# Fourier filter and two dense layers: one way-back matmul instead of two from the ninth group on, with an addition on VectorE and swaps and spreads on ScalarE

## The reference, cut to what matters

```python
X = np.fft.rfft(x, axis=1)                    # x: (2, 3008, 256)
Y = X * (filt_r + 1j * filt_i)[None]
y = np.fft.irfft(Y, n=3008, axis=1).reshape(6016, 256)
h = y @ w_in;  y = elu(h) @ w_out             # w_in (256, 2048), w_out (2048, 256)
h = y @ w2_in; y = (h * clip(h + 3, 0, 6) / 6) @ w2_out
```

## Time and profile before

| | before |
|---|---|
| median of three runs | 1123.72 (1123.43 to 1124.48) |
| the profiled execution's own time | 1124.28 |
| its span | 1122.5 |
| TensorE busy in the span | 1109.4 |
| VectorE, ScalarE, GpSimd busy | 733.0, 761.5, 291.3 |
| granted TensorE clock | 1.0 throughout |

### The profile page before, as it was taken

How to read it: one execution, slowest core, us unless ns; L and a number is a source line. 1 busy time by engine, 2 the same in 40 slices (tenths; PEclk the granted TensorE clock), 3 DMA queues, 4 the chain that set the end, 5 groups by cost and what they waited for, 6 DMA issues and landing times.

```text
span 1122.5 us, 13359 instructions
## 1 busy us (share of the span) xinstructions
PE 1109.4 (99%) x4842; PEld 890.1 (79%) x4842; DVE 733.0 (65%) x900; ACT 761.5 (68%) x1125; POOL 291.3 (26%) x228
## 2 busy tenths in 40 slices
PE   8999899999999999999999999999999999999998
PEld 4666678888888888888888888888888888888886
DVE  6777367566566667566677776666666666665665
ACT  0221588888888888888899766666665666665654
POOL 4876411102102102111269731111111120120000
PEclk9999999999999999999999999999999999999999
DMA  9887300100200200200311200200200101000000
GB/s 256 279 256 226 114 1 1 67 8 1 74 1 1 74 1 1 74 1 1 112 38 57 93 1 1 74 1 1 74 1 24 51 1 37 38 1 1 37 1 37
DMA packets 31185, 59.30 MB, mean 53 GB/s; under 512 B 3600, under 2 KB 19856, under 8 KB 31120
## 3 DMA queue, kind: packets, MB, share of 16 engines
q1 hardware_dynamic: 24784, 48.10, 13.2%
q10 hardware_dynamic: 6336, 10.36, 2.7%
HBM read 39.94 MB, written 18.51 MB: 52 GB/s over the span
## 4 chain that ended last, share of the span: by engine, by line
PE 88%; ACT 6%; DVE 4%; issue 2%; DMA 1%; POOL 0%; ACTq 0%
PE ps L384 41%; PE ps L373 12%; PE ps L375 12%; PE ps L374 12%; PE ps L337 3%; PE ps L312 2%; PE ps L328 2%; PE ps L329 2%; PE ps L320 2%; ACT e L491 2%; DVE e L611 2%; ACT e L493 1%; ACT ystage L485 1%; DMA f_ring<-f_dev 1%; ACT w_hi L467 1%
## 5 line engine op out<-in xcount | busy, mean ns | idle before, releaser
L616 DVE TENSOR_TENSOR g_lo<-e,g_hi 128x502 fp32r<-128x502 f32 (+1 forms) x288 | 277.1, 990 | 135.7 <-ACT g_hi L523 135.7
L373 PE MATMUL ps<-op_hi,w_hi 128*128 128x502 f32 x672 | 262.5, 391 | 2.8 <-ACT ps L518 1.7
L375 PE MATMUL ps<-op_lo,w_hi 128*128 128x502 f32 x672 | 261.8, 390 | 0.0
L374 PE MATMUL ps<-op_hi,w_lo 128*128 128x502 f32 x672 | 261.2, 389 | 0.0
L384 PE MATMUL ps<-g_lo,w_hi 128*128 128x502 f32 x768 | 237.4, 390 | 1.7 <-DVE g_lo L616 1.5
L384 PE MATMUL ps<-g_hi,w_hi 128*128 128x502 f32 x768 | 236.2, 389 | 0.0
L384 PE MATMUL ps<-g_hi,w_lo 128*128 128x502 f32 x768 | 235.6, 388 | 0.0
L682 POOL TENSOR_TENSOR op_lo<-op_raw,op_hi 128x1004 fp32r<-128x1004 f32 (+1 forms) x48 | 100.3, 2091 | 487.9 <-ACT op_hi L475 487.9
L384 PEld LDWEIGHTS ps<-g_lo,w_hi 128*128 128x128 f32 x768 | 143.6, 188 | 33.0 <-DVE g_lo L616 4.4
L384 PEld LDWEIGHTS ps<-g_hi,w_lo 128*128 128x128 f32 x768 | 144.5, 188 | 29.3
L384 PEld LDWEIGHTS ps<-g_hi,w_hi 128*128 128x128 f32 x768 | 144.1, 188 | 29.5 <-ACT g_hi L523 0.6
(11 more groups left out here) (51 smaller groups left out, 1149.8 us busy)
## 6 DMA issues: line engine op xcount, KB each, us to landing
f_ring<-f_dev SPq DMA_DIRECT2D x32, 384.0 KB, 4.4
op_raw<-y SPq DMA_DIRECT2D x36, 251.0 KB, 3.6
x_ring<-x_dev SPq DMA_DIRECT2D x32, 192.0 KB, 4.7
y<-ystage SPq DMA_DIRECT2D x12, 502.0 KB, 2.8
out_dev<-ystage SPq DMA_DIRECT2D x12, 502.0 KB, 2.8
y<-ystage ACTq DMA_DIRECT2D x24, 235.0 KB, 2.8
w_raw<-w_dev ACTq DMA_DIRECT2D x16, 256.0 KB, 4.3
w_raw<-w_dev SPq DMA_DIRECT2D x16, 256.0 KB, 3.1
```

Source lines behind the costliest of these rows:

```text
L373: pe.matmul(out, w_hi[p][:, cols], hi, start=start, stop=False, skip_group_check=True)
L374: pe.matmul(out, w_lo[p][:, cols], hi, start=False, stop=False, skip_group_check=True)
L375: pe.matmul(out, w_hi[p][:, cols], lo, start=False, stop=True, skip_group_check=True).then_inc(done, 1)
L616: return dve.tensor_tensor(g_lo[:, tiles, :], e[:, tiles, :], f32(g_hi[:, tiles, :]), ALU.subtract)
```

## The change

From group 8 on (`NZ`), the imaginary part of the product is no longer carried through a matmul of its own. ScalarE copies the two halves of `part_x` crosswise into a PSUM bank of its own (`swap_halves`, two copies of 64 partitions, bank 1). VectorE multiplies the swapped halves with the signed imaginary filter into `prod_i`, the straight ones with the real filter in place in PSUM, and adds both into `prod_r` (`combine`). One matmul with `I2` remains in `part_r`. The sign of the filter's imaginary part is turned on the host, and `I2J` with it, so that the first eight groups compute what they did. In every second of these groups (odd i) VectorE writes its transposition contiguously into `turned`, and ScalarE spreads it into `back` (`spread`). The inverse pieces have bank 0 alone, and behind the last group bank 2 in turn. TensorE makes `part_x(i + 1)` ahead of `part_a(i + 2)` from step 7 on. The ring of x has seven slots instead of eight; `turned` takes the space.

```diff
--- before.py
+++ after.py
@@ -30,9 +30,11 @@
 IJ = 5
 PIECES = (J + IJ - 1) // IJ
 NPIECE = len(ORDER) * PIECES
-XSLOTS = 8
+LAST_I = NPIECE - PIECES
+XSLOTS = 7
 FSLOTS = 3
 YSLOTS = 4
+NZ = GROUPS
 MATS = ("A", "BX", "I2", "I2J", "I1")
 
 
@@ -88,7 +90,7 @@
             m["BX"][c, 64 + k1], m["BX"][s, 64 + k1] = -si, co
             m["I2"][k1, c], m["I2"][64 + k1, c] = co, -si
             m["I2"][k1, s], m["I2"][64 + k1, s] = si, co
-    m["I2J"][0:64], m["I2J"][64:P] = m["I2"][64:P], -m["I2"][0:64]
+    m["I2J"][0:64], m["I2J"][64:P] = -m["I2"][64:P], -m["I2"][0:64]
     return np.stack([m[n] for n in MATS], axis=1).reshape(P, len(MATS) * P).astype(np.float32)
 
 
@@ -121,6 +123,7 @@
             spec = sbuf(fft, "spec", [P, 2, GCOL])
             prod_r = sbuf(fft, "prod_r", [P, 2, XCOL])
             prod_i = sbuf(fft, "prod_i", [P, 2, XCOL])
+            turned = sbuf(fft, "turned", [P, GCOL])
             back = sbuf(fft, "back", [P, 2, J, P])
         op_hi.append(sbuf(ctx, "op1_hi", [P, 7, T], F32R))
         with ExitStack() as raw:
@@ -140,7 +143,9 @@
             return mats[:, at:at + P]
 
         def ps_i(n):
-            return ps[:, n % 2, 0:IJ * ICOL]
+            return ps[:, 2 if n > LAST_I and (n - LAST_I) % 2 else 0, 0:IJ * ICOL]
+
+        ps_swap = ps[:, 1, 0:XCOL]
 
         def ps_a(i):
             return ps[:, 2 + i % 2, :]
@@ -167,6 +172,8 @@
         zeroed, pad_stored = sem("zeroed"), sem("pad_stored")
         a_done, x_done, r_done, i_done = sem("a_done"), sem("x_done"), sem("r_done"), sem("i_done")
         spec_ready, prod_ready, back_ready = sem("spec_ready"), sem("prod_ready"), sem("back_ready")
+        turn_done, spread_ready = sem("turn_done"), sem("spread_ready")
+        swap_ready, straight_ready, swapped_ready = sem("swap_ready"), sem("straight_ready"), sem("swapped_ready")
         signed = sem("signed")
         i_evac = sem("i_evac")
         y0_stored = [sem(f"y0_stored{k}") for k in range(YSLOTS)]
@@ -191,6 +198,13 @@
 
         def group_of(i):
             return ORDER[i // GROUPS], i % GROUPS
+
+        def direct(i):
+
+            return i < NZ or i % 2 == 0
+
+        def directs(n):
+            return sum(direct(i) for i in range(n))
 
         def piece_at(i):
 
@@ -322,17 +336,26 @@
 
             def part_r(i):
                 pe.wait_ge(prod_ready, i + 1)
-                if i >= 2:
-                    pe.wait_ge(back_ready, i - 1)
+                if i >= 2 and direct(i - 2):
+                    pe.wait_ge(back_ready, directs(i - 1))
+                elif i >= 2:
+                    pe.wait_ge(turn_done, i - 1 - directs(i - 1))
                 dst = ps_r(i)[:, :, 0:K2]
-                pe.matmul(dst, mat("I2"), prod_r[:, i % 2, :], start=True, stop=False)
-                pe.matmul(dst, mat("I2J"), prod_i[:, i % 2, :], start=False, stop=True).then_inc(r_done, 1)
+                if i < NZ:
+                    pe.matmul(dst, mat("I2"), prod_r[:, i % 2, :], start=True, stop=False)
+                    pe.matmul(dst, mat("I2J"), prod_i[:, i % 2, :], start=False, stop=True).then_inc(r_done, 1)
+                else:
+                    pe.matmul(dst, mat("I2"), prod_r[:, i % 2, :], start=True, stop=True).then_inc(r_done, 1)
 
             def part_i(n):
                 pos, j0, nj = piece_cols(n)
-                pe.wait_ge(back_ready, GROUPS * (pos + 1))
-                if n >= 2:
-                    pe.wait_ge(i_evac, n - 1)
+                pe.wait_ge(back_ready, directs(GROUPS * (pos + 1)))
+                if pos:
+                    pe.wait_ge(spread_ready, GROUPS * (pos + 1) - directs(GROUPS * (pos + 1)))
+                if n == LAST_I + 1:
+                    pe.wait_ge(spec_ready, NG - 1)
+                elif n:
+                    pe.wait_ge(i_evac, n - 1 if n > LAST_I else n)
                 for j in range(nj):
                     last = pe.matmul(ps_i(n)[:, j * ICOL:j * ICOL + ICOL], back[:, pos % 2, j0 + j, :],
                                      mat("I1")[:, 0:ICOL], start=True, stop=True)
@@ -353,10 +376,14 @@
             pe.wait_ge(zeroed, 4)
             part_r(0)
             for i in range(1, NG):
-                if i + 2 < NG:
+                if i + 1 < NZ:
                     part_a(i + 2)
-                if i + 1 < NG:
                     part_x(i + 1)
+                else:
+                    if i + 1 < NG:
+                        part_x(i + 1)
+                    if i + 2 < NG:
+                        part_a(i + 2)
                 part_r(i)
                 n = piece_at(i)
                 if n is not None:
@@ -494,10 +521,29 @@
                 else:
                     act.activation(dst, src, ACT.Relu, bias=3.0).then_inc(ready, 1)
 
+            def spread(i):
+                pos, g = i // GROUPS, i % GROUPS
+                act.wait_ge(turn_done, i + 1 - directs(i + 1))
+                if pos >= 2:
+                    act.wait_ge(i_done, PIECES * (pos - 1))
+                act.copy(back[:, pos % 2, :, g * GD:g * GD + GD],
+                         turned[:].rearrange("p (d j) -> p j d", j=J)).then_inc(spread_ready, 1)
+
+            def swap_halves(i):
+                act.wait_ge(x_done, i + 1)
+                if i > NZ:
+                    act.wait_ge(swapped_ready, i - NZ)
+                act.copy(ps_swap[0:64], ps_x(i)[64:P])
+                act.copy(ps_swap[64:P], ps_x(i)[0:64]).then_inc(swap_ready, 1)
+
             for i in range(NG + PIECES):
                 n = piece_at(i - 1) if i <= NG else None
                 if n is not None:
                     evac_piece(n)
+                if NZ <= i + 1 < NG:
+                    swap_halves(i + 1)
+                if 1 <= i <= NG and not direct(i - 1):
+                    spread(i - 1)
                 for p in range(PAIRS):
                     if i == w_step(p) - 2:
                         load_w(p)
@@ -583,13 +629,31 @@
                 dve.tensor_tensor(prod_i[:, i % 2, :], ps_x(i), f_ring[:, i % FSLOTS, 1, :],
                                   ALU.mult).then_inc(prod_ready, 1)
 
+            def combine(i):
+                dve.wait_ge(swap_ready, i - NZ + 1)
+                dve.wait_ge(signed, i + 1)
+                dve.wait_ge(prod_ready, i - 1)
+                dve.wait_ge(r_done, i - 1)
+                dve.tensor_tensor(prod_i[:, i % 2, :], ps_swap, f_ring[:, i % FSLOTS, 1, :],
+                                  ALU.mult).then_inc(swapped_ready, 1)
+                dve.wait_ge(f_loaded[i % FSLOTS], 16 * (i // FSLOTS + 1))
+                dve.tensor_tensor(ps_x(i), ps_x(i), f_ring[:, i % FSLOTS, 0, :], ALU.mult).then_inc(straight_ready, 1)
+                dve.wait_ge(swapped_ready, i - NZ + 1)
+                dve.wait_ge(straight_ready, i - NZ + 1)
+                dve.tensor_tensor(prod_r[:, i % 2, :], ps_x(i), prod_i[:, i % 2, :], ALU.add).then_inc(prod_ready, 1)
+
             def turn_r(i):
                 pos, g = i // GROUPS, i % GROUPS
                 dve.wait_ge(r_done, i + 1)
                 if pos >= 2 and g == 0:
                     dve.wait_ge(i_done, PIECES * (pos - 1))
                 dst = back[:, pos % 2, :, g * GD:g * GD + GD].rearrange("p j d -> p d j")
-                dve.transpose(dst, ps_r(i)).then_inc(back_ready, 1)
+                if direct(i):
+                    dve.transpose(dst, ps_r(i)).then_inc(back_ready, 1)
+                else:
+                    if directs(i) < i:
+                        dve.wait_ge(spread_ready, i - directs(i))
+                    dve.transpose(turned[:], ps[:, 6 + i % 2, :]).then_inc(turn_done, 1)
 
             dve.memset(back[:, 0, 0:4, :], 0.0).then_inc(zeroed, 1)
             dve.memset(pad_zero[:], 0.0).then_inc(zeroed, 1)
@@ -601,8 +665,10 @@
             for i in range(NG):
                 if i + 2 < NG:
                     turn_a(i + 2)
-                if i + 1 < NG:
+                if i + 1 < NZ:
                     products(i + 1)
+                elif i + 1 < NG:
+                    combine(i + 1)
                 turn_r(i)
 
             def second_act(u, src, ap, ready, done):
@@ -732,7 +798,7 @@
         rows = f[row].reshape(N1, K2, DH, GROUPS, GD).transpose(2, 0, 3, 4, 1)
         parts.append(np.concatenate([rows, rows], axis=1).reshape(DH, P, GROUPS, XCOL))
     f_dev = np.concatenate(parts, axis=3).transpose(0, 1, 2, 3)
-    sign_dev = np.concatenate([sgn, sgn], axis=0)
+    sign_dev = np.concatenate([-sgn, sgn], axis=0)
 
     def pieces(w_in, w_out):
         a = w_in.reshape(DH, P, PAIRS, 2, P).transpose(2, 1, 0, 3, 4)
```

## The result

The changed kernel takes 1126.95 us (median of 16 runs, 1124.13 to 1128.96) against 1123.99 of the kernel before: a ratio of 1.0024, 95% interval 1.0017 to 1.0031. It is slower by 3.0 us, where 1119.3 us was predicted. Its profiled execution is its fastest run, 1124.13, with a span of 1122.3.

A forecast was written before the change was run, and what follows sets the result against it. The weight-load ring was taken to bound the stage: 37.67 + 10.9 + 11.2 + 30.3 = 90.1 us, last X 110.4, tail 6.1, last pieces 116.5 not 120.89. 1124.28 - 4.4 = 1119.9 profiled, 1119.3 median; range 1113.0 to 1125.0.

The forecast's parts named there:

- The step that failed: Behind the start of the last pieces, pieces and dense layers keep their length, so the 4.4 us gain stays.
- the tail: From the last X product to the last seven pieces: 6.1 us, against 5.01 before, with pieces starting at 116.5.
- rival (c): Weight loads land slower as DMA has little room: 1126.3 us at 1.4 us more, 1129.3 at 2 more; chance 0.12.
- TensorE's step: In the transform stage, a step with a piece falls from 3.91 to 3.27 us without the second way-back matmul.
- VectorE: Its work per new-way group takes 2.85 us on the mean, under 3.27, so it does not bound piece steps.
- the swap: Two ScalarE copies from PSUM to PSUM, 466 ns each, 0.87 us for both, bounds 0.75 and 1.1.
- The spread: ScalarE's copy of 512 columns in SBUF: 0.62 us, 0.55 with overlap, 0.95 kept as the dearer case.
- rival (b): Copies and spreads on ScalarE are dearer, swap 1.1 us and spread 0.95: 1123.0 us; chance 0.18.
- The ring: Three-step loop of weight rounding, load issue, landing and GpSimd's sums sets the pace: 10.9, 11.2, then 10.1 us a block.
- Rival (a): TensorE sets the stage's pace and the ring costs nothing after block 2: 1113.4 us; chance 0.20.
- The block ends: In the one step of eight without a piece, VectorE becomes the bound, at 0.5 us each.
- The start: DMA-bound opening: one x slot less brings the rounding of block 2 forward 0.65 us, to 37.67.

The follow-up runs named there:

- e9: Changed kernel without spreads, last two groups the old way, and each weight load issued only after the swap ahead of it completed: 1117.19 us, ratio 0.9939.

## Why the prediction was wrong

**The step that failed** is the sentence that all behind the last pieces' start "has the same instructions and is carried along". The instructions are the same, but not their clock: 12.62 - 7.38 = 5.24 us on the last pieces and 3.21 - 1.88 = 1.33 on the four behind them, 6.6 us together. The waits that did it were in the sum: the tail was called "a chain with nothing beside it", its length was worked out, and the question of what an idle TensorE does was not put. None of the rivals had it. That the median lies near the 1126.3 us of rival (c) is chance.

For the profiled executions the sum closes. 1119.9 us was predicted and 1124.13 measured, 4.2 more: 6.6 of clock, less 1.4 because the last pieces started at 115.08 and not at 116.5, less 0.9 because from the first matmul of the dense layers to the end of the span it is 992.2 us, against 993.1 before. The prediction had named a change of this last length as a sign of its being wrong. It is not the change's: three other kernels here have 992.2 too (the one without spreads, the same with filled waits, and e9), the rest 993.0 to 993.4, and no run says why. The median lies 2.8 us above the profiled run, in part for the clock, as told above.

With the tail filled the changed kernel measured 1119.9, where 1119.3 was predicted. That is partly luck: the errors of the other steps, which follow, cancel in part, and in that kernel's trace the last pieces start at 117.45.

**TensorE's step, VectorE, the swap: right.** 3.27 us in piece steps, and VectorE below it. Its timeline in a step:

```profile
73.52 0.52 DVE L637 TENSOR_TENSOR prod_i<-ps,f_ring 128x384 f32<-128x384 f32 x1
73.96 0.56 DVE L640 TENSOR_TENSOR ps<-ps,f_ring 128x384 f32<-128x384 f32 x1
74.62 0.56 DVE L643 TENSOR_TENSOR prod_r<-ps,prod_i 128x384 f32<-128x384 f32 x1
75.10 0.71 DVE L656 STREAM_TRANSPOSE turned<-ps 128x512 f32<-128x512 f32 x1
```

From start to start it is 0.44 + 0.66 + 0.48 us. The addition waits for its own engine and starts 0.66 us after the product ahead of it, which is that product's 0.56 and 0.10 more: the upper bound of the prediction, where 0.60 was taken. Lines by form (busy us, mean ns, idle ahead of them):

```profile
L643 DVE TENSOR_TENSOR prod_r<-ps,prod_i 128x384 f32<-128x384 f32 x24 | 13.4, 558 | 2.5
L640 DVE TENSOR_TENSOR ps<-ps,f_ring 128x384 f32<-128x384 f32 x24 | 13.3, 556 | 0.0
...
L529 ACT COPY back<-turned 128x512 f32<-128x512 f32 x12 | 13.2, 1100 | 1.6 <-DVE turned L656 1.6
...
L536 ACT COPY ps<-ps 64x384 f32<-64x384 f32 x24 | 10.8, 452 | 11.9 <-PE ps L334 9.3 <-ACT ystage L486 1.8 <-DVE prod_i L637 0.7
```

A product written to PSUM takes 556 ns, one written to SBUF 558, so the bounds of the prediction were wider than needed. A swap copy is 452 ns against 466.

**The spread: wrong by size.** 1100 ns against 620 taken, and above the upper bound of 0.95 us. Spreads above 0.8 us were a sign of rival (b), whose other half, dearer swaps, did not come. The Trainium skill's rule on SBUF cachelines (SBUF — State Buffer, Specifications (TRN2)) had pointed there: each cross to a new 16-byte line pays a penalty. The trace agrees with it: the rounding of 502 columns in a row takes 0.61, the spread of 512, read with a step of 128 bytes, 1.10. That the step alone did it is argued and not shown: the spread also writes in runs of 16 numbers, and no run has a copy of this size in a row.

**The ring: wrong in its first term, right in its place.** ScalarE's timeline in the changed kernel:

```profile
37.24 1.37 ACT L494 CAST w_hi<-w_raw 128x1408 fp32r<-128x1408 f32 x1 [2.92 <-POOL w_raw L722]
...
39.52 0.45 ACT L536 COPY ps<-ps 64x384 f32<-64x384 f32 x1 [0.46 <-ACT ystage L486]
39.62 0.33 ACTq L478 DMA_DIRECT2D w_raw<-w_dev  x1
...
46.10 1.37 ACT L494 CAST w_hi<-w_raw 128x1408 fp32r<-128x1408 f32 x1
...
87.18 1.37 ACT L494 CAST w_hi<-w_raw 128x1408 fp32r<-128x1408 f32 x1 [1.41 <-POOL w_raw L722]
```

The weight load is issued at 39.62, 0.10 us after the first copy of the swap started: so it did not wait for the swap to finish, as the prediction had assumed. From rounding 2 to the second issue it is 2.74 us, as in the earlier trace rows (2.70) without a swap. And rounding 3 starts 8.86 us after rounding 2, not 10.9, so the landing was at most 4.3 us, not 5.4 (the profile has 3.9 for its second load). Roundings 2 and 7 are 49.9 us apart; 52.4 was predicted. Blocks 3 to 6 show no wait for GpSimd at all, where the prediction wanted waits at least as long as before. Rival (a) was nearer for this stretch. In the sum of the prediction itself block 7 comes to 5.47 + 4.1 = 9.6 us and not 9.7; nothing hangs on it, since 10.1 was taken.

**The block ends: wrong by size.** 0.5 us was given to a step without a piece. TensorE's timeline at the ends of the second and third column block:

```profile
61.65 0.91 PE L348 MATMUL ps<-prod_r,mats 128*128 128x384 f32 x2 [0.43 <-DVE prod_r L643]
63.44 1.32 PE L360 MATMUL ps<-mats,back 128*128 128x94 f32 x10 [0.88 <-issue]
...
90.59 1.32 PE L360 MATMUL ps<-mats,back 128*128 128x94 f32 x10 [1.32 <-issue]
```

From the short piece (56.04) to the next full one (63.44) it is 7.40 us; before it was 65.72 - 59.68 = 6.04, and with two products less it should be 4.75. So 2.65 us are lost at each of the two inner block ends, not 0.5: swap, three VectorE operations and a spread stand in a row there. Without spreads it is 6.87 and 6.40 us, so the spread is 0.5 and 1.0 us of the loss, and the larger part remains without it.

**The start and the tail.** Rounding 2 came 1.08 us earlier (0.65 taken). One pair of traces does not measure this term: in the kernels that share the changed kernel's text up to there, piece 0 starts anywhere from 33.21 to 35.78 us (34.93 in the changed kernel, 36.21 before). The tail from the last X to the pieces took 115.08 - 108.10 = 6.98 us, 6.1 was predicted; the spread is 0.55 of the difference. The errors up to the last pieces are small and cancel in part: the start -0.4, rounding 2 to rounding 7 -2.5, rounding 7 to the last X +0.6 (87.18 to 108.10, where 90.1 to 110.4 was predicted), the tail +0.9. Their sum is the -1.4 between 115.08 and the predicted 116.5.

**Rival (c)**, a slower landing, did not happen on the mean. The second loads of blocks 3 to 7 (L452 before, L479 after) took 5.4, 5.2, 4.5, 4.0 and 4.1 us before and 3.9, 5.1, 4.4, 5.0 and 5.0 after: the first came 1.5 us sooner, the last two 0.9 to 1.0 later.

## What to carry to other kernels

Before an edit takes work from TensorE where it then waits, ask what its clock does behind the wait, and read the granted clock by windows on both sides of it: here 1.3 us of matmuls saved in the last two groups cost over 6 us in those that follow. Where a chain over other engines can't be shortened, put matmuls whose output nobody reads into the wait, or leave the short old way for the last groups. They gave 7.0 and 9.4 us, and the change with its waits filled is worth some 4 (1119.9 against 1124.3). And move work from an engine only where that engine is late: the spreads relieved VectorE, which had time, and cost 2.1 to 2.7 us by the medians, 1.3 and 1.6 in two pairs of traces.

## What the runs showed of the hardware

- The granted clock of TensorE fell to 0.5 (1.2 GHz) behind waits of 1.61 and 1.96 us with one product of 0.9 us between them, and in another kernel, with the same wait of 1.93 us behind 2.7 us of matmuls, in four runs of six. It did not fall behind 1.26 and 1.15 us, and in the kernel before not behind a single wait of 1.67 us (at 20.71 us, [1.67 <-DVE prod_i L583]). The length of one wait does not decide it, and the runs do not say what does.
- It then stayed at 0.5 to the end of the last pieces, while TensorE was busy throughout with matmuls of 94 columns and their weight loads, which run at full clock where the clock had not fallen: 12.62 us in the changed kernel and 13.65 to 13.97 in three others, against 7.38. The Trainium skill (TensorE: Matmul & The Clock Gate, The HAM clock gate) describes two levels and a rise under sustained work. The two levels are here; of the rise these traces say otherwise, for in all four it came only with the matmuls of 502 columns behind the pieces. At 40 us, among the stage's mixed work, the clock was back after some 3.4 us. Why the one rises late and the other soon is open.
- ScalarE's queue issues a DMA while a copy ahead of it still runs (at 39.62 us, 0.10 after the start of the first of two copies of 0.45 each).
- A VectorE instruction that waits for the one ahead of it on its own engine starts 0.66 us after it, and one without such a wait 0.44 to 0.48 after it.
